# Pooling one pair ahead on GpSimd, and the local mask as an identity product on TensorE

## The chip, the cores and the metric

The kernel runs on one core of one Trainium2 chip. The metric is the time of one execution on the device, in microseconds. The core has TensorE (matrix products into the accumulator banks, PSUM), VectorE, ScalarE, GpSimd (which does not touch PSUM here) and SyncE, whose queue SP issues the loads and stores.

## The reference

Inputs are q, k and v of shape (2, 8, 576, 64), the weights of one feed-forward layer (512 to 2048 to 512) and of four experts (512 to 1024 to 512), and the experts' probabilities for 1152 tokens.

```python
# attention, per batch and head, S = 576, D = 64, factor 4
q_d, k_d, v_d = means over 4 neighbouring positions      # 144 positions
out_up = repeat(softmax(q_d k_d^T / 8) v_d, 4)
mask = abs(i - j) < 4
out_local = softmax(where(mask, q k^T / 8, -1e9)) v
x = (out_up + out_local) as (1152, 512)
h = x @ w_in;  x = (h * sigmoid(h)) @ w_out
p = probs / (probs.sum(-1) + 1e-9)
out = sum over e of p[:, e] * (relu(x @ w1[e]) @ w2[e])
```

## The kernel before, in words

The 16 heads are worked on as N = 8 pairs; the two heads of a pair lie in partitions 0 to 63 and 64 to 127. A software pipeline over `s` runs `step(s)` on each engine; `stage(n, do)` does the part of pair n if it exists. The order within a step is written out by hand for each engine, and semaphores join the engines. A query block has 32 rows (18 blocks a head), and only the window of 38 keys around it is computed: `scores` (L695) makes 36 small products a pair into two banks (`SLB`), `scores_down` (L712) four products of the pooled q and k.

TensorE's step (L766) is: `scores(s)`, `turn_p0(s-1)`, `scores_down(s)`, `values(s-2)`, `turn_p1(s-1)`. The turns (L672, L682; the instructions are at L664 and L669) transpose the probabilities, `values` (L723; L736 local, L743 pooled) multiplies them by v. `warm(count)` (L659) issues transposes whose result nobody reads, ahead of and within the first steps.

VectorE's step (L585): the mask is added to the local scores in place, in PSUM (`mask_scores`, L527, L533), then the row maximum (L537), the subtraction (L542), the pooled maximum (L549), the sums and the normalisation (`norm_local`, L552, which writes `pl` at L565; `norm_down`), and `final(s-2)`, which writes the pair's result `xf`. ScalarE's step (L431) moves the turned probabilities out of PSUM (`evac_p1`, `evac_pd`, `evac_p0`), takes the exponentials (`exp_local` L401, `exp_down`), copies the pooled output (`evac_up`, L421), rounds a pair's result to `x_hi` (`x_high`, L427) and a unit of weights to `wa_hi` (`split_hi`, L366).

GpSimd's step (L327): `down_qk(s)` (L294) adds neighbours of q and k, for q at L300 and L305, for k at L309 and L312; `down_v(s-1)` (L282) does it for v; `x_low` (L314) and `low_unit` (L319) make the rests of x and of a weight unit, `x_lo` and `wa_lo`. `scores(n+1)` needs `pl` of pair n, since it writes the banks that pair n's scores held; `scores_down(n)` needs `qd` and `kd` of pair n; `down_qk` of a pair needs that `scores_down` of the one before has read them.

SP's step (L233) loads q and k of pair s+1 (after `scores` and the pooling of pair s-1), v of pair s, the windows of v of pair s-1 (after `values` of pair s-3), and at s = 0, 1, 3 and 5 a unit of weights. `EARLY` (L179) says in which step a unit is split into its two parts.

After the pairs come the two layers, each product as three (high by high, high by low, low by high) with the data of the two parts. Layer one's first tiles (L757, L796) already run between the last pairs' `values`.

Of the kernel before, what the change touches and what calls it, by code (L numbers as in the profile page):

```python
# [14 lines left out]
P = 128  # L15
# [10 lines left out]
def program(nc, qk, vw, vr, w, probs, out, dims):  # L26
# [31 lines left out]
    with ExitStack() as ctx:  # L58
# [117 lines left out]
            if 0 <= n < N:  # L176
                do(n)

        EARLY = {1: 0, 2: 1, 3: 2, N: 3}  # L179
        XHALF = N // 2  # L180

        def x_of(x, n):
# [21 lines left out]
        @block.sync  # L204
        def _(sp):
            def load_qk(n):
                if n >= 2:
                    sp.wait_ge(s_full, n - 1)
                    sp.wait_ge(qkd_ready, 2 * n - 2)
                sp.dma_start(qk_raw[:, n % 2, :], qk[n]).then_inc(qk_in[n % 2], 16)  # L210

            def load_v(n):
                if n >= 2:
                    sp.wait_ge(vd_ready, n - 1)
                sp.dma_start(v_raw[:, n % 2, :, :, :].rearrange("p a r d -> p (a r d)"), vr[n])\
                    .then_inc(v_in[n % 2], 16)

            def load_win(n):
                if n >= 2:
                    sp.wait_ge(pv_done, n - 1)  # L220
                for h in range(2):
                    sp.dma_start(v_win[HS * h:HS * h + ROWS, n % 2, :, :].rearrange("p g d -> p (g d)"), vw[n, h])\
                        .then_inc(vw_in[n % 2], 16)

            def load_unit(slot, src):
                sp.dma_start(w_raw[:, slot, :], src).then_inc(raw_in[slot], 16)

            def early_unit(u):
                if u >= RAW:
                    sp.wait_ge(w_ready, u - RAW + 1)  # L230
                load_unit(u % RAW, w[u])

            def step(s):  # L233
                stage(s + 1, load_qk)
                stage(s, load_v)
                stage(s - 1, load_win)
                if s in (0, 1):
                    early_unit(s)
                if s in (3, 5):
                    early_unit((s + 1) // 2)  # L240
                if s == 3:
                    sp.dma_start(pr[:, :, :].rearrange("p t e -> p (t e)"), probs).then_inc(pr_in, 16)

            load_qk(0)
            for s in range(N + 1):
                step(s)
            with sp.Fori(2, (FT1 + E * FT2) // RAW) as i:
                for s in range(RAW):
                    u = i * RAW

                    sp.wait_ge(w_ready, u + s - RAW + 1)
                    load_unit(s, w[bass.ds(u + s, 1)].rearrange("o p n -> p (o n)"))
            with sp.Fori(0, T // P) as t:

                sp.wait_ge(out_done, t + (E * (T // P) + 1))
                sp.dma_start(out_v[bass.ds(t, 1)].rearrange("o p d -> p (o d)"),
                             o_acc[:, bass.ds(t, 1), :].rearrange("p o d -> p (o d)")).then_inc(pr_in, 16)
            sp.wait_ge(pr_in, 16 * (1 + T // P))

        @block.gpsimd  # L260
        def _(pool):
# [63 lines left out]
                                   ALU.subtract).then_inc(w_ready, 1)  # L325

            def step(s):  # L327
                stage(s, down_qk)
                stage(s - 1, down_v)
                if s - 4 in range(XHALF):  # L330
                    x_low(s - 4)
                if s in EARLY:
                    u = EARLY[s]
                    low_unit(u + 1, slice(u, u + 1), areas[0], u % RAW)

            for s in range(N + 1):
                step(s)

            def low_units(u0, area, skip=0):
# [22 lines left out]
        def _(act):  # L362
# [68 lines left out]
            def step(s):  # L431
                if s == N + 1:
                    hidden1(0, 0)
                stage(s - 2, evac_p1)
                stage(s - 2, evac_pd)
                stage(s - 1, evac_p0)
                stage(s, exp_local)
                stage(s, exp_down)
                if s == N:
                    act.wait_ge(tick_set, 1)  # L440
                    act.activation(tick[:, 3:4], tick[:, 0:1], ACT.Silu)
                if s == N + 1:
                    hidden1(1, 1)
                stage(s - 2, evac_up)
                if s - 4 in range(XHALF):
                    x_high(s - 4)
                if s in EARLY:
                    split_hi(EARLY[s])

# [52 lines left out]
        def _(dve):  # L502
            dve.memset(ident[:, :], 0.0).then_inc(zeroed, 1)
            dve.memset(band[:, :], 0.0).then_inc(zeroed, 1)
            dve.memset(pl[:, :, :, 0, W:HS], 0.0).then_inc(zeroed, 1)
            odd = GQ * (G % QP)
            dve.memset(ps[odd:P, SLB:SLB + 2, (GT - 1) * W:LC], 0.0).then_inc(zeroed, 1)
            DSTEPS = 5

            def own(n, k):  # L510
                return n * DSTEPS + k
# [12 lines left out]
            def scores_view():  # L524
                return local_scores(0, LC).rearrange("p h (t j) -> p h t j", j=W)

            def mask_scores(n):  # L527
                dve.wait_ge(s_full, n + 1)
                if n == 0:
                    dve.wait_ge(mask_set, QP + 2)  # L530
                    dve.wait_ge(zeroed, 4)
                m = mask[:, :, :].rearrange("p t j -> p (t j)").unsqueeze(1).to_broadcast([P, 2, LC])
                dve.tensor_tensor(local_scores(0, LC), local_scores(0, LC), m, ALU.add).then_inc(dve_step, 1)  # L533

            def max_local(n):
                dve.wait_ge(dve_step, own(n, 1))
                dve.tensor_reduce(mx[:, :].rearrange("p (h t) -> p h t", h=2), scores_view(), AX.X, ALU.max)\  # L537
                    .then_inc(dve_step, 1)

            def sub_max(n):  # L540
                dve.wait_ge(dve_step, own(n, 2))
                dve.tensor_tensor(scores_view(), scores_view(), per_score(mx), ALU.subtract).then_inc(sub_done, 1)  # L542

            def max_down(n):
# [7 lines left out]
            def norm_local(n):  # L552
                par = n % 2
                dve.wait_ge(exp_done, n + 1)
                total = ps[:, SLB, LC:LC + 2 * GT]
                dve.tensor_reduce(total.rearrange("p (h t) -> p h t", h=2), scores_view(), AX.X, ALU.add)\
                    .then_inc(dve_step, 1)
                dve.wait_ge(dve_step, own(n, 3))
                dve.tensor_scalar(rse[:, :], total, EPS, None, ALU.add).then_inc(dve_step, 1)
                dve.wait_ge(dve_step, own(n, 4))  # L560
                dve.reciprocal(rr[:, :], rse[:, :]).then_inc(dve_step, 1)
                dve.wait_ge(dve_step, own(n, 5))
                if n >= 2:
                    dve.wait_ge(p1_turned, n - 1)
                dve.tensor_tensor(pl[:, par, :, :, 0:W].rearrange("p t h j -> p h t j"), scores_view(), per_score(rr),  # L565
                                  ALU.mult).then_inc(pl_ready, 1)
# [16 lines left out]
                    .then_inc(xf_done, 1)  # L583

            def step(s):  # L585
                stage(s, mask_scores)
                stage(s, max_local)
                stage(s, sub_max)
                stage(s, max_down)
                stage(s, norm_local)  # L590
                stage(s, norm_down)
                stage(s - 2, final)
                if s == N:
                    hidden1(0, 0)
# [63 lines left out]
        def _(pe):  # L658
# [36 lines left out]
            def scores(n):  # L695
                par = n % 2
                pe.wait_ge(qk_in[par], 16 * (n // 2 + 1))
                if n >= 1:
                    pe.wait_ge(pl_ready, n)
                else:  # L700
                    pe.wait_ge(zeroed, 4)
                for g in range(G):
                    t, c = g // QP, g % QP
                    at = t * W
                    for h in range(2):
                        rows = slice(D * h, D * h + D)
                        ins = pe.matmul(ps[GQ * c:GQ * c + GQ, SLB + h, at:at + W],
                                        qk_raw[rows, par, GQ * g:GQ * g + GQ],
                                        qk_raw[rows, par, S + GQ * g:S + GQ * g + W], start=True, stop=True)
                ins.then_inc(s_full, 1)  # L710

            def scores_down(n):  # L712
# [48 lines left out]
            def in1(blk, f):  # L761
                layer_in(tile1(blk, f), blk, f, *areas[f // HALF], f)

            WARM = (8, 3, 6, 5, 3)

            def step(s):  # L766
                if s == N + 1:
                    in1(0, 1)
                stage(s, scores)
                if s == 0:  # L770
                    warm(WARM[1])
                stage(s - 1, turn_p0)
                stage(s, scores_down)
                if s < 2:
                    warm(WARM[2 + s])
                stage(s - 2, values)
                if s == N:
                    pe.wait_ge(xlo_done, XHALF)
                    pe.wait_ge(expd_done, 4 * N)
                    in1(0, 0)  # L780
                stage(s - 1, turn_p1)
# [102 lines left out]
```

## Time and profile before

| | us |
|---|---|
| median of 3 runs | 710.99 (710.86 to 712.01) |
| the profiled execution | 711.14 |
| its span, first to last instruction | 709.3 |
| TensorE busy | 685.5 (97%) |
| VectorE, ScalarE, GpSimd busy | 199.5, 163.4, 163.8 |
| `scores` of pair 0 and of pair 7 start at | 4.21 and 75.51 |
| end of the last `values` | 102.53 |

The page cuts the span into 40 slices of 17.7 us; digits are the busy share in tenths, and PEclk is the granted clock in tenths of full speed. Durations of matmuls are modelled at their end, so the distance between the starts of two blocks is the better price of a block. A group's line in the timeline gives start, length, engine, line and operation, shapes and count, and in brackets the idle time before it and what ended that.

### The profile page before, as it was taken

Reading aid. Unit: us, or ns where it says so; the run is one execution under the profiler, and the core shown is the slowest. Engines: PE = TensorE matmul, PEld = TensorE weight load, DVE = VectorE, ACT = ScalarE, POOL = GpSimd, SP = SyncE. Lnnn points to the kernel's source line nnn. Section 1 sums busy time; section 2 is a strip of 40 time slices with the busy share of each in tenths; the row PEclk is TensorE's granted clock in tenths of the full one; section 3 lists DMA queues with packets and bytes.
Section 4 is the critical chain, followed back from the end, with each engine's and each line's share of the span. In section 5 each row is a group of like instructions: output and inputs, shape, how many; then the busy total and the mean of one; then the engine's idle time right before and its main releaser. Section 6 shows DMA issues by size and latency. Waiting matters only on the chain.

```text
span 709.3 us, 11721 instructions
## 1 busy us (share of the span) xinstructions
PE 685.5 (97%) x4574; PEld 635.2 (90%) x4574; DVE 199.5 (28%) x348; ACT 163.4 (23%) x337; POOL 163.8 (23%) x115
## 2 busy tenths in 40 slices
PE   7788899899999999999999999999999999999997
PEld 5577799899999999998989899999999998989896
DVE  7445426733222322221212212121212121212211
ACT  4344443322111213343101042111241111101010
POOL 4636437750000004556000064000262000000000
PEclk9555569999999999999999999999999999999999
DMA  9544213330000001334000033000040000001001
GB/s 272 135 125 132 70 55 119 120 119 1 0 1 1 0 0 65 131 100 149 30 0 0 0 119 118 0 0 0 28 149 0 0 0 0 0 0 44 18 27 44
DMA packets 11227, 38.58 MB, mean 54 GB/s; under 512 B 1536, under 2 KB 1536, under 8 KB 11200
## 3 DMA queue, kind: packets, MB, share of 16 engines
q1 hardware_dynamic: 11200, 38.19, 17.0%
q8 instruction: 20, 0.33, 0.2%
q14 instruction: 7, 0.06, 0.0%
HBM read 35.83 MB, written 2.36 MB: 54 GB/s over the span
## 4 chain that ended last, share of the span: by engine, by line
PE 85%; issue 7%; POOL 5%; DMA 1%; DVE 1%; ACT 0%; DVEq 0%; POOLq 0%; SPq 0%; ACTq 0%
PE ps L757 41%; PE ps L812 28%; PE ps L796 13%; PE ps L736 1%; POOL v L287 1%; POOL x_lo L316 1%; POOL wa_lo L323 1%; POOL k L309 1%; POOL vd L292 1%; POOL q L300 1%; DMA qk_raw<-qk 0%; DMA w_raw<-w 0%; PE ps L743 0%; POOL qd L305 0%; DVE g_lo L601 0%
## 5 line engine op out<-in xcount | busy, mean ns | idle before, releaser
L623 DVE SCALAR_TENSOR_TENSOR g_lo<-ps,g_hi 128x384 fp32r<-128x384 f32 x96 | 53.5, 558 | 270.5 <-ACT g_hi L461 270.5
L461 ACT ACTIVATE g_hi<-ps 128x384 fp32r<-128x384 f32 x96 | 47.1, 491 | 299.8 <-PE ps L757 299.7
L323 POOL TENSOR_TENSOR wa_lo<-w_raw,wa_hi 128x1024 f32 (+1 forms) x24 | 57.3, 2393 | 240.5 <-ACT wa_hi L364 240.4
L757 PE MATMUL ps<-x_hi,wa_hi 128*128 (+1 forms) x288 | 97.4, 338 | 0.0
L757 PE MATMUL ps<-x_hi,wb_hi 128*128 (+1 forms) x288 | 97.2, 337 | 0.0
L757 PE MATMUL ps<-x_lo,wb_hi 128*128 (+1 forms) x288 | 97.1, 337 | 0.0
L757 PE MATMUL ps<-x_hi,wa_lo 128*128 (+1 forms) x288 | 97.1, 337 | 0.0
L757 PE MATMUL ps<-x_hi,wb_lo 128*128 (+1 forms) x288 | 97.0, 337 | 0.0
L757 PE MATMUL ps<-x_lo,wa_hi 128*128 (+1 forms) x288 | 96.9, 336 | 0.0
L323 POOL TENSOR_TENSOR wb_lo<-w_raw,wb_hi 128x1024 f32 x24 | 57.8, 2416 | 104.8 <-ACT wb_hi L364 104.6
L599 DVE CAST g_hi<-g_act 128x384 fp32r<-128x384 f32 x48 | 29.9, 622 | 120.6 <-ACT g_act L456 120.6
L812 PE MATMUL ps<-wa_hi,g_lo 128*128 128x512 f32 x144 | 56.7, 394 | 0.0
L812 PE MATMUL ps<-wb_hi,g_lo 128*128 128x512 f32 x144 | 56.7, 394 | 0.0
L812 PE MATMUL ps<-wa_lo,g_hi 128*128 128x512 f32 x144 | 56.7, 394 | 0.0
L812 PE MATMUL ps<-wb_lo,g_hi 128*128 128x512 f32 x144 | 56.4, 391 | 0.0
L757 PEld LDWEIGHTS ps<-x_hi,wa_hi 128*128 128x128 f32 x288 | 54.6, 190 | 1.9 <-issue 0.4
L812 PE MATMUL ps<-wb_hi,g_hi 128*128 128x512 f32 x144 | 56.3, 391 | 0.0
L812 PE MATMUL ps<-wa_hi,g_hi 128*128 128x512 f32 x144 | 56.0, 389 | 0.0
L757 PEld LDWEIGHTS ps<-x_lo,wa_hi 128*128 128x128 f32 x288 | 54.5, 189 | 1.5
L757 PEld LDWEIGHTS ps<-x_lo,wb_hi 128*128 128x128 f32 x288 | 54.2, 188 | 1.6
L757 PEld LDWEIGHTS ps<-x_hi,wb_hi 128*128 128x128 f32 x288 | 54.3, 189 | 1.4
L757 PEld LDWEIGHTS ps<-x_hi,wa_lo 128*128 128x128 f32 x288 | 54.4, 189 | 0.0
(95 smaller groups left out, 969.4 us busy)
## 6 DMA issues: line engine op xcount, KB each, us to landing
w_raw<-w SPq DMA_DIRECT2D x48, 512.0 KB, 3.5
qk_raw<-qk SPq DMA_DIRECT2D x8, 579.0 KB, 4.5
v_win<-vw SPq DMA_DIRECT2D x16, 216.0 KB, 3.9
v_raw<-vr SPq DMA_DIRECT2D x8, 288.0 KB
out<-o_acc SPq DMA_DIRECT2D x9, 256.0 KB, 2.0
pr<-probs SPq DMA_DIRECT2D x1, 18.0 KB, 4.4
```

The costliest lines, as they stand in the source:

```text
L287: pool.tensor_tensor(v2[:, :, :, :], v_raw[:, par, :, 0:2, :], v_raw[:, par, :, 2:4, :], ALU.add)\
L292: pool.tensor_tensor(vd[:, par, :, :], v2[:, :, 0, :], v2[:, :, 1, :], ALU.add).then_inc(vd_ready, 1)
L300: pool.tensor_tensor(q2[:, :], qv[:, :, 0], qv[:, :, 1], ALU.add).then_inc(qk2_done, 1)
L309: pool.tensor_tensor(k2[:, :], kv[:, :, 0], kv[:, :, 1], ALU.add).then_inc(qk2_done, 1)
L316: pool.tensor_tensor(x_of(x_lo, n), xf[:, n, :], x_of(x_hi, n).bitcast(F32), ALU.subtract).then_inc(xlo_done, 1)
L323: pool.tensor_tensor(lo[:, at, :].rearrange("p o n -> p (o n)"), w_raw[:, s, :], hi[:, at, :].rearrange("p o n -> p (o n)").bitcast(F32), ...
L461: act.activation(g_hi[:, f % GB, :], ps[:, HB + f % 4, 0:NB], ACT.Relu).then_inc(relu_done, 1)
L599: dve.tensor_copy(g_hi[:, f % GB, :], g_act[:, f % 2, :]).then_inc(ghi_done, 1)
L623: dve.scalar_tensor_tensor(out=g_lo[:, f % GB, :], in0=ps[:, HB + f % 4, 0:NB], scalar=0.0, in1=g_hi[:, f % GB, :].bitcast(F32), op0=ALU.m ...
L757: ins = pe.matmul(dst, w[:, f % HALF, c], x[:, kt, at], start=(kt == 0 and i == 0), stop=(kt == KT - 1 and i == 2))
L796: ins = pe.matmul(ps[:, ACCB + j, 0:NB], w[:, f % HALF, c], g[:, f % GB, :], start=(f == 0 and i == 0), stop=(f == FT1 - 1 and i == 2))
L812: ins = pe.matmul(ps[:, ACCB + j, 0:DM], g[:, f % GB, c], w[:, f % HALF, KT * P:UNIT], start=(f == 0 and i == 0), stop=(f == FT2 - 1 and i ...
```

## The change

GpSimd pools pair 0 ahead of the loop and pair s+1 in step s; its loop has one step more, and its `low_unit` of `EARLY` comes one step later than ScalarE's `split_hi`. `EARLY` has step 4 where it had 3, and SP loads these units in steps 4 and 6. ScalarE rounds a pair's result one step earlier. TensorE starts each pair's local scores with two products of the identity by the mask (128 x 190, one for each head's bank), which open the accumulation; the 36 small products add to it. VectorE's mask pass and the memset of the unused part of the banks are gone. In TensorE's step `scores_down(s)` comes ahead of `turn_p0(s-1)`, and the counts of warm-up transposes grow.

```diff
-        EARLY = {1: 0, 2: 1, 3: 2, N: 3}
+        EARLY = {1: 0, 2: 1, 4: 2, N: 3}
...
-                if s in (3, 5):
-                    early_unit((s + 1) // 2)
+                if s in (4, 6):
+                    early_unit(s // 2)
...
             def step(s):
-                stage(s, down_qk)
+                stage(s + 1, down_qk)
                 stage(s - 1, down_v)
                 if s - 4 in range(XHALF):
                     x_low(s - 4)
-                if s in EARLY:
-                    u = EARLY[s]
+                if s - 1 in EARLY:
+                    u = EARLY[s - 1]
                     low_unit(u + 1, slice(u, u + 1), areas[0], u % RAW)
 
-            for s in range(N + 1):
+            down_qk(0)
+            for s in range(N + 2):
                 step(s)
...
-                if s - 4 in range(XHALF):
-                    x_high(s - 4)
+                if s - 3 in range(XHALF):
+                    x_high(s - 3)
...
-            odd = GQ * (G % QP)
-            dve.memset(ps[odd:P, SLB:SLB + 2, (GT - 1) * W:LC], 0.0).then_inc(zeroed, 1)
-            DSTEPS = 5
+            DSTEPS = 4
...
-            def mask_scores(n):
-                dve.wait_ge(s_full, n + 1)
-                if n == 0:
-                    dve.wait_ge(mask_set, QP + 2)
-                    dve.wait_ge(zeroed, 4)
-                m = mask[:, :, :].rearrange("p t j -> p (t j)").unsqueeze(1).to_broadcast([P, 2, LC])
-                dve.tensor_tensor(local_scores(0, LC), local_scores(0, LC), m, ALU.add).then_inc(dve_step, 1)
-
             def max_local(n):
-                dve.wait_ge(dve_step, own(n, 1))
+                dve.wait_ge(s_full, n + 1)
...
                 if n >= 1:
                     pe.wait_ge(pl_ready, n)
                 else:
-                    pe.wait_ge(zeroed, 4)
+                    pe.wait_ge(mask_set, QP + 2)
+                for h in range(2):
+                    pe.matmul(ps[:, SLB + h, 0:LC], ident[:, :], mask[:, :, :].rearrange("p t j -> p (t j)"),
+                              start=True, stop=False, skip_group_check=True)
...
                                         qk_raw[rows, par, GQ * g:GQ * g + GQ],
-                                        qk_raw[rows, par, S + GQ * g:S + GQ * g + W], start=True, stop=True)
+                                        qk_raw[rows, par, S + GQ * g:S + GQ * g + W], start=False, stop=True,
+                                        skip_group_check=True)
...
-            WARM = (8, 3, 6, 5, 3)
+            WARM = (12, 4, 12, 8, 5)
 
             def step(s):
                 if s == N + 1:
                     in1(0, 1)
+                if s == 2:
+                    warm(WARM[4])
                 stage(s, scores)
                 if s == 0:
                     warm(WARM[1])
-                stage(s - 1, turn_p0)
                 stage(s, scores_down)
                 if s < 2:
                     warm(WARM[2 + s])
+                stage(s - 1, turn_p0)
                 stage(s - 2, values)
```

## Rows read from the trace of the kernel before

**Rows 1.** The page: granted clock in 40 slices.

```profile
PEclk9555569999999999999999999999999999999999
```

**Rows 2.** Busy time by stretch: stretch, length, engines, clock, DMA share, GB/s.

```profile
15.56:29.11 13.55, 9.73 (x174) 8.08 (x174) 6.78 (x15) 5.94 (x20) 6.42 (x7) 0.57 0.53 137
53.36:64.43 11.07, 9.75 (x174) 8.20 (x173) 5.69 (x12) 4.54 (x18) 5.43 (x8) 0.50 0.59 168
75.51:87.31 11.80, 9.82 (x174) 8.20 (x174) 5.69 (x12) 5.16 (x19) 6.16 (x8) 0.50 0.22 58
```

**Rows 3.** TensorE's waits up to 103 us: total, times, longest.

```profile
PE ps L719 <- POOL kd L312: 11.8, 6, 2.6
```

**Rows 4.** Timeline of TensorE, pair 6's step.

```profile
64.44 1.08 PE L707 MATMUL ps<-qk_raw 64*32 64x38 f32 x72
65.45 1.09 PE L664 MATMUL ps<-ident,pl 128*102 128x128 f32 x4
67.86 1.24 PE L719 MATMUL ps<-kd,qd 64*72 64x144 f32 x8 [1.32 <-POOL kd L312]
69.03 4.05 PE L736 MATMUL ps<-plT,v_win 38*64 38x32 f32 x72
73.01 1.23 PE L743 MATMUL ps<-pdT,vd 72*64 72x144 f32 x8
74.16 0.46 PE L664 MATMUL ps<-ident,pl 128*102 128x128 f32 x1
75.51 0.44 PE L707 MATMUL ps<-qk_raw 64*32 64x38 f32 x24
```

**Rows 5.** Timeline of GpSimd in the same step.

```profile
64.14 1.41 POOL L316 TENSOR_TENSOR x_lo<-xf,x_hi 128x576 fp32r<-128x576 f32 x1 [5.40 <-ACT x_hi L364]
67.38 0.42 POOL L312 TENSOR_TENSOR kd<-k 128x144 f32<-128x144 f32 x1
```

**Rows 6.** Timeline of TensorE: blocks at the higher clock.

```profile
33.84 0.72 PE L719 MATMUL ps<-kd,qd 64*72 64x144 f32 x8 [2.63 <-POOL kd L312]
34.49 0.74 PE L736 MATMUL ps<-plT,v_win 38*64 38x32 f32 x10
...
96.81 0.27 PE L664 MATMUL ps<-ident,pl 128*102 128x128 f32 x1
...
97.38 0.42 PE L757 MATMUL ps<-x_hi,wa_hi 128*128 128x384 f32 x1
...
99.67 2.29 PE L736 MATMUL ps<-plT,v_win 38*64 38x32 f32 x72
101.88 0.71 PE L743 MATMUL ps<-pdT,vd 72*64 72x144 f32 x8
102.53 0.47 PE L796 MATMUL ps<-g_hi,wa_hi 128*128 128x384 f32 x1
```

**Rows 7.** Timeline of VectorE: the mask pass.

```profile
65.55 0.56 DVE L533 TENSOR_TENSOR ps<-ps,mask 128x380 f32<-128x380 f32 x1 [1.27 <-PE ps L707]
```

**Rows 8.** Timeline of TensorE and ScalarE in step 1.

```profile
11.77 1.24 PE L719 MATMUL ps<-kd,qd 64*72 64x144 f32 x8
14.17 0.67 PE L669 MATMUL ps<-ident,pd 72*72 72x72 f32 x8
15.59 0.35 PE L707 MATMUL ps<-qk_raw 64*32 64x38 f32 x26 [0.76 <-DVE pl L565]
...
13.32 0.47 ACT L404 ACTIVATE ps<-ps 128x380 f32<-128x380 f32 x1 [0.85 <-DVE ps L542]
```

**Rows 9.** Busy time by stretch: at two changes of the granted clock.

```profile
31.20:31.40 0.20, 0.01 (x1) 0.00 (x0) 0.17 (x1) 0.15 (x1) 0.20 (x1) 1.00 0.67 123
102.60:102.80 0.20, 0.20 (x1) 0.20 (x2) 0.00 (x0) 0.16 (x1) 0.00 (x0) 1.00 0.00 0
102.80:103.00 0.20, 0.20 (x2) 0.20 (x2) 0.04 (x1) 0.20 (x2) 0.00 (x0) 0.50 0.00 0
```

**Rows 10.** The chain that ended last, from 95 us: its piece after the last values.

```profile
102.64 0.03 ACT up L364
```

More of the change, by code:

```diff
@@ L525, in scores_view, with max_local @@
                 return local_scores(0, LC).rearrange("p h (t j) -> p h t j", j=W)
-            def mask_scores(n):
+            def max_local(n):
                 dve.wait_ge(s_full, n + 1)
-                if n == 0:
-                    dve.wait_ge(mask_set, QP + 2)
-                    dve.wait_ge(zeroed, 4)
-                m = mask[:, :, :].rearrange("p t j -> p (t j)").unsqueeze(1).to_broadcast([P, 2, LC])
-                dve.tensor_tensor(local_scores(0, LC), local_scores(0, LC), m, ALU.add).then_inc(dve_step, 1)
-            def max_local(n):
-                dve.wait_ge(dve_step, own(n, 1))
                 dve.tensor_reduce(mx[:, :].rearrange("p (h t) -> p h t", h=2), scores_view(), AX.X, ALU.max)\
@@ L540, in sub_max @@
             def sub_max(n):
-                dve.wait_ge(dve_step, own(n, 2))
+                dve.wait_ge(dve_step, own(n, 1))
                 dve.tensor_tensor(scores_view(), scores_view(), per_score(mx), ALU.subtract).then_inc(sub_done, 1)
@@ L557, in norm_local @@
                     .then_inc(dve_step, 1)
+                dve.wait_ge(dve_step, own(n, 2))
+                dve.tensor_scalar(rse[:, :], total, EPS, None, ALU.add).then_inc(dve_step, 1)
                 dve.wait_ge(dve_step, own(n, 3))
-                dve.tensor_scalar(rse[:, :], total, EPS, None, ALU.add).then_inc(dve_step, 1)
+                dve.reciprocal(rr[:, :], rse[:, :]).then_inc(dve_step, 1)
                 dve.wait_ge(dve_step, own(n, 4))
-                dve.reciprocal(rr[:, :], rse[:, :]).then_inc(dve_step, 1)
-                dve.wait_ge(dve_step, own(n, 5))
                 if n >= 2:
@@ L585, in step @@
             def step(s):
-                stage(s, mask_scores)
                 stage(s, max_local)
```

## The prediction

> **What bounds the kernel now.** I read the page first: one core, a span of 709.3 us, 711.14 with what lies around it, and a granted TensorE clock that is low in slices 5 to 9 alone [rows 1]. From about 130 us on TensorE is full at the higher level, and the change does not touch that part. So the question is the attention, up to the last `values` product near 102.5 us.
>
> I then cut the attention at the starts of `scores`, with a view of busy time by stretch [rows 2]. A step is one pair of heads. Pair 2's takes 13.55 us, pair 5's 11.07 us, pair 7's 11.80 us up to the turn at 87.31. In pair 5's step TensorE is busy 9.75 us of 11.07, VectorE 5.69, GpSimd 5.43, all at clock 0.50, the lower of TensorE's two levels (1.2 GHz; the higher is 2.4). TensorE bounds the step, and it has a hole.
>
> The view of waits names the hole: `scores_down` waited for GpSimd's pooling of k, 11.8 us in 6 waits, at most 2.6 [rows 3].  The timeline of one step shows why [rows 4, 5]: GpSimd does `x_low` first, whose `x_hi` copy stands in ScalarE's queue behind `evac_up`, the end of the previous pair's `values`; only then it pools, until 67.80, while TensorE could have started at 66.4. With `low_unit` (2.4 us) in the place of `x_low` (1.41) the hole is 2.6 us.
>
> The prices of TensorE's blocks follow from the starts in this step, at the lower level [rows 4]: `scores` 65.45 - 64.44 = 1.01; `turn_p0` 1.0; `scores_down` 69.03 - 67.86 = 1.17; `values`, local part, 73.01 - 69.03 = 3.98, pooled part 74.16 - 73.01 = 1.15; `turn_p1` 75.51 - 74.16 = 1.35. Sum 9.66. At the higher level the same blocks are [rows 6]: `scores_down` 34.49 - 33.84 = 0.65; `values` 101.88 - 99.67 = 2.21 and 102.53 - 101.88 = 0.65; `turn_p1` 97.38 - 96.81 = 0.57; `turn_p0` half of 1.0, estimated 0.5. `scores` is 72 tiny products whose rate I hold for the same at both levels, 1.0. Sum 5.6. So the clock is worth 4.1 us a step, three times the hole.
>
> **The change, part by part.** *Pooling ahead.* GpSimd pools pair s+1 in step s, after `scores_down(s)` has read `qd` and `kd`. Its work in a step is 5.43 us [rows 2], and `x_low` now takes an `x_hi` that ScalarE wrote a step before, so GpSimd waits for nothing late. SP's load of pair n, which waited for the pooling of n-2, may go earlier; the loads of v and of its windows keep their waits. One more pair of `low_unit` moves goes with it; they stay beside TensorE. Gain: the hole, 2.6 us in steps 2 to 4 and 1.3 in 5 to 7, all of it. What would be late next is TensorE's own work.
>
> *The mask.* VectorE loses one pass, 0.56 us and its gap, 0.6 us [rows 7], which lies in the chain from `scores` to `pl` and not on TensorE's path after step 2. TensorE gains two products of 128x128 by 190 columns per pair, in fp32, each issued as two instructions. None is in the trace. The nearest rows are `scores_down`, eight instructions of 144 columns in 1.17 us. If the two row halves (h = 0, 1) run beside each other, one instruction has 0.29 us for 144 columns, and the mask's four cost 4 x 0.29 x 190/144 = 1.5 us; if they run in turn it is 0.77. Four transposes of 128 columns in 1.0 us give 4 x 0.25 x 190/128 = 1.5 too, so I take 1.5 at the lower and 0.8 at the higher level, with 0.77 as the low end and, should the identity's loads not hide (four loads near 0.17 us), 2.2 as the high end. All of it is on the path. With it a step of TensorE's is 9.66 + 1.5 = 11.15 us at the lower level and 5.6 + 0.8 = 6.4 at the higher. So if the clock stays, the mask eats what the pooling gives in steps 5 to 7 (11.07 before): the change lives by the clock. The dropped VectorE memset lies in TensorE's warm-up and costs nothing either way; the new wait for `mask_set` ends at about 3.4 us, before the q and k load lands at 4.2.
>
> *The order.* `turn_p0(s-1)` goes behind `scores_down(s)`. On ScalarE `evac_p0(s-1)` waits for it, and `exp_local(s)` stands behind that, then VectorE's sums and `pl`, for which `scores(s+1)` waits. From the exponential's start to the next `scores` it is 15.59 - 13.32 = 2.3 us [rows 8]. At the higher level `pl` is there at 0.8 + 1.0 + 0.65 + 0.5 + 0.7 (evacuation) + 2.3 = 5.95 us, just inside 6.4; at the lower at 7.7 of 11.15. Covered, except in steps 0 and 1, which have no `values` to cover it.
>
> *Steps 0 and 1, and the warm-up products.* Twelve transposes at 0.25 us end at 4.6 instead of before 4.21, the mask ends at 6.1, `scores(0)` at 7.1 against 5.2, less VectorE's 0.6: step 1 would start 1.3 us later at the lower level, less if the clock has risen; I take 0.8 later, 10.5. In step 1 the exponential waits for mask, `scores`, `scores_down`, eight warm products, `turn_p0` and the evacuation: 6.65 + 0.7 + 2.3 = 9.7 us at the lower, 7.0 at the higher level, against 5.85 before. I take 8.0: step 2 starts at 18.5 instead of 15.56. Loss 2.9 us.
>
> The duration rows tell more of this start than the clock column, which says 1.00: `scores_down` takes 1.24 us at 11.77, as at the lower level, and the turn of eight tiles 0.67 at 14.17, as at the higher [rows 4, 6, 8]. So the clock rose only near 14 us, and fell before 20.
>
> *The clock.* In the old kernel it stood at 1.00 at 31.2 us, after slices at half speed [rows 1, 9], right after `turn_p1`, `scores` and `turn_p0` had run without a hole. It fell at 102.8 with TensorE busy all through both sides [rows 9]: behind it lay `values`, small tiles. The new step holds both kinds: `turn_p1`, mask, `scores`, `scores_down`, `turn_p0` in one block of 1.35 + 1.5 + 1.0 + 1.2 + 1.0 = 6 us with the densest product of all in it, then 5 us (2.9 at the higher level) of `values`. So I expect a rise in the first half of every step and a fall in or after the second, and take the mean of the two prices: (11.15 + 6.4) / 2 = 8.8 us.
>
> Sum: 18.5 + 6 x 8.8 = 71.3 us for the turn of pair 7, against 87.31: 16 us less. What follows (15.2 us to the end of the last `values`, then a chain that begins with that pair's `up` copy at 102.64 [rows 10]) is the same work in the same order and moves as a whole. Against the profiled execution's 711.14: 711.1 - 16.0 = 695.1. The median of the runs shown is 710.99, so the same forecast holds for it.
>
> The Trainium skill's page "TensorE: Matmul & The Clock Gate", section on PE-mode transpose, says that transposes do not count as busy for the clock. By that the warm products would be worth nothing, steps 0 and 1 would run at the lower level, step 2 would start at 21.3 and the sum would be 698. The rows speak against it: the rise near 14 us came after turns, `scores_down` and five warm transposes.
>
> **Rivals.** *A: the clock rises and stays (chance 0.11).* For it: no hole is left. Against: the fall at 102.8 with TensorE busy. Steps of 6.4 us from 17.0: 55.4 at pair 7's turn, 31.9 us less, and some 3 more from the tail: 676. The same page's practical advice has the clock fall back for idle gaps alone; by that rule the new kernel would do just this.
>
> *B: the clock stays low; the mask on TensorE is the new bound (0.13).* For it: in the old trace it stayed at 0.50 through all of pairs 5 to 7 with 9.75 of 11.07 us busy [rows 2], and TensorE was without a hole from 67.86 to 76.5 [rows 4]. Against: the rise near 31. Step 2 starts at 21.3, six steps of 11.15 end at 88.2, 0.9 later than 87.31: 712. The mask's price decides: at 0.77 us it would be 706, at 2.2 some 717; above 1.35 us this rival is slower than before. This is the case on the other side.
>
> *The forecast (0.76)* has its own range from the share of a step at the higher level: 8.8 +- 1.2 us, 688 to 702.
>
> **Numbers.** 0.2% is 1.4 us, about what a measurement of this kernel can tell from no change. The forecast and A are faster (0.87); B is split by the mask's price, 0.08 slower, 0.04 within, 0.01 faster. The range 680 to 709 leaves out most of A below and B's upper half above, some 2 in 10.
>
> **What would show it.** `scores_down` waits for GpSimd no more; two new products of 190 columns stand ahead of `scores`, some 0.75 us each at the lower level; the line of VectorE's mask is gone; steps of 8 to 10 us with the clock changing inside each, `values` some times 2.2 us and some times 4. Pair 7's turn near 71 us, and the work from there on unchanged. I am wrong if the steps are above 10 us (B), below 7 (A), or if a new wait stands on TensorE: for `pl` after step 1, or for a load of q and k.

## The result and the profile after

The changed kernel takes 693.68 us (median of 4 runs, 692.11 to 694.59) against 710.92 for the kernel before, a ratio of 0.9752 with a 95% interval of 0.9728 to 0.9776. The forecast was 695. A second comparison on another chip gave 693.61 and 0.9744 (0.9716 to 0.9773). The runs of the changed kernel scatter by up to six us, those of the kernel before by up to three, apart from one execution beside experiments 1 to 4 that took 842.6 us at a mean clock of 0.73, a slow state that is not compared.

The profiled execution took 694.59 us, its span is 692.7. The page, which answers to [rows 1]:

```profile
span 692.7 us, 11813 instructions
PEclk9857899999999999999999999999999999999999
```

The low digits are fewer and uneven: the clock now changes inside the attention. The view of busy time by stretch, cut at the start of each pair's first mask product, pair 2 to pair 7, answers to [rows 2] (columns as there: stretch, length, TensorE, its weight loads, VectorE, ScalarE, GpSimd, clock, DMA share, GB/s):

```profile
16.33:22.66 6.33, 6.33 (x178) 5.45 (x178) 5.52 (x13) 4.80 (x17) 4.80 (x8) 1.00 0.63 151
22.66:33.48 10.82, 8.65 (x181) 7.35 (x178) 9.97 (x12) 5.06 (x18) 8.41 (x9) 0.77 0.75 186
33.48:44.52 11.04, 11.04 (x179) 9.31 (x178) 8.51 (x13) 4.47 (x17) 7.14 (x9) 0.50 0.70 192
44.52:52.88 8.36, 8.36 (x180) 6.91 (x178) 4.26 (x8) 4.83 (x17) 4.30 (x6) 0.70 0.43 120
52.88:62.81 9.93, 9.10 (x179) 7.69 (x178) 9.32 (x14) 4.70 (x18) 9.59 (x10) 0.67 0.65 157
62.81:71.47 8.66, 7.80 (x180) 6.49 (x178) 6.37 (x13) 4.55 (x18) 4.58 (x5) 0.81 0.29 73
```

Here both of my bounds stand as whole steps: 6.33 us with the clock high throughout (forecast 6.4), 11.04 with it low throughout (forecast 11.15), TensorE without a hole in either. The others lie between. VectorE's column is new as well: 5.69 to 6.78 us a step before, up to 9.97 now, with no more instructions.

TensorE's largest waits up to 90 us, in place of [rows 3]:

```profile
PE ps L693 <- DVE pl L556: 2.2, 2, 1.2
PE ps L700 <- issue: 2.2, 1, 2.2
...
PE ps L654 <- ACT pdT L365: 0.9, 1, 0.9
PE ps L730 <- DVE xf L573: 0.8, 1, 0.8
```

The 11.8 us of waiting for GpSimd's pooled k are gone. The waits for `pl` end steps 0 and 1. The one called issue (the engine waited for nothing that the profile shows) is a hole in pair 3's step, and the one for `xf`, in pair 6's, is new.

The timeline of TensorE, first pair 1, then pair 4's step, gives the price of the product that [rows 4] could not show:

```profile
9.78 0.88 PE L693 MATMUL ps<-mask,ident 128*128 128x190 f32 x4 [0.99 <-DVE pl L556]
10.60 0.84 PE L700 MATMUL ps<-qk_raw 64*32 64x38 f32 x72
11.37 0.71 PE L713 MATMUL ps<-kd,qd 64*72 64x144 f32 x8
...
33.48 1.57 PE L693 MATMUL ps<-mask,ident 128*128 128x190 f32 x4
34.98 1.08 PE L700 MATMUL ps<-qk_raw 64*32 64x38 f32 x72
35.98 1.24 PE L713 MATMUL ps<-kd,qd 64*72 64x144 f32 x8
```

From start to start the product takes 0.82 us at the higher level and 1.50 at the lower; `scores` takes 0.77 and 1.00.

The last pair's `up` copy, the head of the chain after the attention, stood at 102.64 [rows 10] and is now, in the chain that ended last, here:

```profile
86.11 0.03 ACT up L365
```

That is 16.5 us earlier, and the span is 16.6 us shorter. All of the gain is in the attention, and what follows moved as a whole.

### The profile page after: what moved, and what is told of

Same layout as the page of the kernel before. It is cut to its first block, busy times and chain, and to the rows that moved or that the text cites. A ratio compares the mean times of both kernels' runs of the same rounds, so it can differ in the third digit from the quotient of the medians.

```text
span 692.7 us, 11813 instructions
## 1 busy us (share of the span) xinstructions
PE 677.3 (98%) x4625; PEld 628.9 (91%) x4625; DVE 207.3 (30%) x339; ACT 162.2 (23%) x337; POOL 165.1 (24%) x115
## 4 chain that ended last, share of the span: by engine, by line
PE 93%; DVE 2%; POOL 2%; issue 1%; ACT 1%; DMA 0%; DVEq 0%; POOLq 0%; SPq 0%; ACTq 0%
PE ps L751 42%; PE ps L808 29%; PE ps L792 13%; PE ps L730 3%; PE ps L693 1%; PE ps L654 1%; PE ps L737 1%; POOL x_lo L316 1%; PE ps L700 1%; PE ps L713 1%; POOL wa_lo L323 1%; PE ps L651 1%; PE ps L659 1%; DVE rsde L562 1%; DMA w_raw<-w 0%
```

## The experiments

Each was run beside the kernel before, and ratios are to it. Line numbers are those of each kernel's own file.

**1. The mask back on VectorE, all else of the change kept.** The pass and the memset come back, the product goes.

```diff
-                for h in range(2):
-                    pe.matmul(ps[:, SLB + h, 0:LC], ident[:, :], mask..., start=True, stop=False, ...)
...
-                ... start=False, stop=True, skip_group_check=True)
+                ... start=True, stop=True)
...
+                stage(s, mask_scores)
                 stage(s, max_local)
```

> The changed kernel with the mask back on VectorE and the identity product gone; all else of the change stays. Theory (the dense product is what lifts the clock): TensorE's step is 9.66 us at the lower level and 5.6 at the higher, but the clock rises in fewer steps; steps of about 9 us, pair 7's turn near 73 us, some 695 to 698 us, no faster than the changed kernel. Rival (the product is only a cost, the clock alternates without it): steps of (9.66 + 5.6) / 2 = 7.6 us, 686 to 688 us.

Measured: 693.45 us (691.68 to 694.49), 0.9742 (0.9718 to 0.9767): the same as the changed kernel. The rival's 686 to 688 is out. The theory's main point holds, that taking the product away makes the kernel no faster, though its time was 2 to 4 us too long.

**2. The pooling ahead alone.** The kernel before, with this, the longer loop and the later weight units:

```diff
-                stage(s, down_qk)
+                stage(s + 1, down_qk)
...
-                if s in EARLY:
-                    u = EARLY[s]
+                if s - 1 in EARLY:
+                    u = EARLY[s - 1]
...
+            down_qk(0)
...
-                if s - 4 in range(XHALF):
-                    x_high(s - 4)
+                if s - 3 in range(XHALF):
+                    x_high(s - 3)
```

> The kernel before with only the pooling ahead (and what goes with it on SP, ScalarE and in GpSimd's loop); old order, old warm-up, mask on VectorE. Theory: the hole goes in all six steps, at least 12 us saved, 697 to 699 if the clock stays low and about 690 if it rises in every other step. Rival (the hole was a symptom, another wait takes its place): over 705.

Measured: 696.67 us, 0.9793 (0.9775 to 0.9810), and no wait for the pooled k is left. A pair's step from its timeline of TensorE, up to the next one's `scores`:

```profile
26.88 1.08 PE L708 MATMUL ps<-qk_raw 64*32 64x38 f32 x72
27.89 1.09 PE L665 MATMUL ps<-ident,pl 128*102 128x128 f32 x4
28.91 1.24 PE L720 MATMUL ps<-kd,qd 64*72 64x144 f32 x8
30.08 4.05 PE L737 MATMUL ps<-plT,v_win 38*64 38x32 f32 x72
34.06 1.23 PE L744 MATMUL ps<-pdT,vd 72*64 72x144 f32 x8
...
36.56 0.69 PE L708 MATMUL ps<-qk_raw 64*32 64x38 f32 x38
```

The step is 36.56 - 26.88 = 9.68 us, the 9.66 of [rows 4] with the hole cut out, all at the lower level. The pooling by itself carries 2.1% of the 2.5%. Between this kernel and that of experiment 1, run beside the same kernel before, lie only the order of the turns and the warm-up counts, and the intervals are apart (696.67 and 693.45 us). So what the change gives beyond the pooling is there without the mask product.

**3. The mask product alone.** The kernel before, with VectorE's pass and the memset gone and the two products in `scores`.

```diff
+                for h in range(2):
+                    pe.matmul(ps[:, SLB + h, 0:LC], ident[:, :], mask[:, :, :].rearrange("p t j -> p (t j)"),
+                              start=True, stop=False, skip_group_check=True)
...
-                stage(s, mask_scores)
```

> The kernel before with only the mask as an identity product on TensorE, VectorE's pass gone; GpSimd pools as before. Theory: the product, 1.50 us at the lower level, goes ahead of scores, while GpSimd's chain is what TensorE waits for in scores_down; the hole of 1.3 to 2.6 us hides most of it, and the clock rises more often: 705 to 711. Rival (the product lies on the path and the clock does not follow): 6 x 1.5 less the holes, over 713.

Measured: 704.29 us, 0.9909 (0.9880 to 0.9938), a little faster than I had allowed. Its TensorE waits less for the pooled k, though the longest wait is 3.2 us, not 2.6:

```profile
PE ps L712 <- POOL kd L312: 6.8, 4, 3.2
```

6.8 us instead of 11.8 [rows 3]: the product fills part of the hole, and the mean granted clock from 20 to 70 us is 0.67 instead of 0.53. Parts 2 and 3 add up to 3.0%, the whole change gives 2.5%, which the intervals hardly tell apart. With the hole gone the product gives nothing more: experiment 1.

**4. The old counts of warm-up transposes.**

```diff
-            WARM = (12, 4, 12, 8, 5)
+            WARM = (8, 3, 6, 5, 3)
```

> The changed kernel with the old counts of warm-up transposes (8, 3, 6, 5, 3). Theory: the clock is at the higher level from about 5 us in the changed kernel; with fewer transposes it rises later or falls within steps 0 to 2, which costs 2 to 5 us: 695 to 699. Rival (the transposes do not count for the clock and only fill time): no difference or up to 1 us faster, 692 to 694.

Measured: 695.04 us, 0.9771 (0.9742 to 0.9800). The centre is where the theory had it, but the interval overlaps the changed kernel's. In its profile `scores_down` of pair 0 already runs at the higher level (7.57 to 8.25 us), where the old kernel's took 1.24 us at 6.04; in the changed kernel the higher level stands at `scores` of pair 0, 5.25 us. That is not the counts alone: in the first profile of experiment 8, with the same step 0 as the changed kernel, `scores` still takes 1.02 us at 5.76.

**5. Transposes among the values products.**

```diff
                 for turn_over in range(2):
+                    for _ in range(3):
+                        pe.transpose(ps[:, OUTB, 3 * P:4 * P], ident[:, :], ident[:, :])
                     for i in range(G // 2):
```

> The changed kernel with 2 x 3 transposes of the identity (128 columns each, result unread) among each pair's local values products. They cost 1.5 us a step at the lower and 0.8 at the higher level. Theory (it is the small tiles of values that let the clock fall, TensorE busy or not): the clock stays high through most steps, 6.4 + 0.8 = 7.2 us a step, pair 7's turn near 60 us, 682 to 687. Rival (the fall has another cause): the transposes are pure cost, 7 or 8 pairs by 1.15, some 701 to 703.

Measured: 698.03 us, 0.9807 (0.9786 to 0.9828). Neither number came. Three transposes take 0.42 to 0.47 us at the higher level in its timeline, so six in each of eight pairs cost at least 7 us, and about 4 are seen (the intervals allow 1.6 to 6.2). A part comes back, and by the time alone it cannot be said whether from the clock.

**6. The mask product twice.**

```diff
-                for h in range(2):
+                for h in (0, 1, 0, 1):
                     pe.matmul(ps[:, SLB + h, 0:LC], ident[:, :], mask...
```

> The changed kernel with the mask product issued twice per bank (the second overwrites the first with the same values). Theory (the product pays for itself in clock): of the 1.5 or 0.8 us more a step a good part comes back, 694 to 699. Rival (pure cost): 8 pairs by 1.15 us, 702 or more.

Measured: 695.55 us (692.17 to 697.13), 0.9768 (0.9731 to 0.9806). Pure cost is out: at least 0.64 us more per pair at the higher level and 1.26 at the lower, eight times, would be 5 to 10 us, and 2 are seen (the intervals allow up to 4.3).

**7. The mask product in bf16.**

```diff
-        mask = asb("mask", [P, GT, W])
+        mask = sb("mask", [P, GT, W], BF16, att)
+        ident16 = sb("ident16", [P, P], BF16, att)
...
-                    pe.matmul(ps[:, SLB + h, 0:LC], ident[:, :],
+                    pe.matmul(ps[:, SLB + h, 0:LC], ident16[:, :],
```

> The changed kernel with mask and identity in bf16 for the mask product, one instruction instead of two for each bank; 0 and the large negative value are as good in it. The product should cost at most 0.4 us a pair at the lower level instead of 1.50. Theory (what is saved in columns is lost in clock): 690 to 695, as with the mask on VectorE. Rival (pure cost): 1.1 us at the lower, 0.6 at the higher level saved, 685 to 688.

Measured: 694.28 us, 0.9785 (0.9740 to 0.9830). In the timeline the cheap product takes 0.45 us at the lower and 0.26 at the higher level, against 1.50 and 0.82, and the kernel gains nothing by it. Its view of busy time over three steps points to why:

```profile
26.00:56.00 30.00, 29.90 (x524) 25.23 (x526) 21.81 (x35) 13.90 (x49) 20.56 (x23) 0.50 0.68 173
```

TensorE is busy 29.90 us of 30 and is granted 0.50 all the time. The changed kernel in the same stretch:

```profile
26.00:56.00 30.00, 29.57 (x538) 24.90 (x539) 22.45 (x33) 13.82 (x49) 20.38 (x23) 0.60 0.64 164
```

It is no busier, and has more clock; the bf16 kernel of experiment 10 has 0.50 in this stretch as well. What the two differ in is the product, dense and long in the one and short in the other. The granted clock from 20 to 70 us, in the same view, through kernels with less and more of it. Pooling ahead only:

```profile
20.00:70.00 50.00, 48.84 (x948) 41.49 (x947) 44.77 (x68) 25.75 (x92) 37.66 (x39) 0.57 0.58 149
```

Mask on VectorE:

```profile
20.00:70.00 50.00, 45.87 (x892) 38.10 (x888) 43.63 (x68) 26.21 (x94) 37.08 (x40) 0.62 0.65 167
```

The changed kernel:

```profile
20.00:70.00 50.00, 47.00 (x945) 39.71 (x942) 39.14 (x61) 24.98 (x92) 35.80 (x38) 0.69 0.61 154
```

Transposes among the values products:

```profile
20.00:70.00 50.00, 46.21 (x907) 38.41 (x903) 37.59 (x55) 22.46 (x81) 35.41 (x38) 0.76 0.60 154
```

The product twice:

```profile
20.00:70.00 50.00, 44.62 (x1063) 38.64 (x1063) 38.74 (x62) 25.43 (x91) 37.20 (x40) 0.90 0.63 159
```

The first profile of experiment 8, which has the same dense product as the changed kernel:

```profile
20.00:70.00 50.00, 44.25 (x987) 36.88 (x986) 35.67 (x65) 26.78 (x97) 36.50 (x40) 0.82 0.68 166
```

In this view the two kernels without the product have 0.57 and 0.62, the two with it in bf16 (experiments 7 and 10) 0.66 and 0.63, and the seven with one fp32 product between 0.67 and 0.82. The transposes among the `values`, at 0.76, are inside that spread; the product twice, at 0.90, is above it. TensorE's busy time lies between 43.85 and 48.84 us in all of them and does not order them.

These are single profiles. The mean clock over the whole execution is known for every run, and orders the kernels alike:

| | runs | mean clock, lowest to highest |
|---|---|---|
| pooling ahead only (experiment 2) | 4 | 0.949 to 0.966 |
| mask on VectorE (1) | 4 | 0.956 to 0.968 |
| product in bf16 (7, 10) | 9 | 0.949 to 0.968 |
| changed kernel, both times | 10 | 0.964 to 0.980 |
| `final` first, both times (8) | 9 | 0.966 to 0.983 |
| old order (9) | 5 | 0.962 to 0.980 |
| old warm-up counts (4) | 4 | 0.926 to 0.973 |
| transposes among the `values` (5) | 4 | 0.975 to 0.978 |
| product twice (6) | 4 | 0.981 to 0.985 |

The product alone with the old pooling (experiment 3) has 0.953 to 0.966, where the kernel before has mostly 0.936 to 0.945. The attention is an eighth of the execution, so the differences are small: by my estimate 0.01 is 14 us (0.02 of 691) more or less at the lower level. Not every one of these means fits its time (three runs of the kernel before have 1.00 at 711 to 713 us), so only groups count.

**8. VectorE's `final(s-2)` ahead of `norm_down(s)`.** The new wait for `xf` led here. In the changed kernel's timeline of VectorE and of GpSimd, pair 5's step:

```profile
51.99 3.72 DVE L562 TENSOR_SCALAR rsde<-rsd 72x4 f32<-72x4 f32 x1
...
55.96 0.97 DVE L566 TENSOR_TENSOR pd<-pd,rrd 72x576 f32<-72x576 f32 x1
56.85 0.74 DVE L573 TENSOR_TENSOR xf<-ps,up 128x576 f32<-128x576 f32 x1
...
51.97 1.41 POOL L316 TENSOR_TENSOR x_lo<-xf,x_hi 128x576 fp32r<-128x576 f32 x1
53.34 2.35 POOL L323 TENSOR_TENSOR wa_lo<-w_raw,wa_hi 128x1024 fp32r<-128x1024 f32 x1
```

An addition on 72 x 4 values, 0.17 us in the old kernel, takes 3.72: it begins as GpSimd's `x_low` does and ends with its `low_unit`. In pair 2's step it is the `pd` product, 3.47 us instead of 0.75. VectorE's `xf` stands behind them, and `values` waits for `xf`.

```diff
-                stage(s, norm_down)
-                stage(s - 2, final)
+                stage(s - 2, final)
+                stage(s, norm_down)
```

> The changed kernel with VectorE's final(s-2) ahead of norm_down(s). In the changed kernel the pd product of norm_down takes up to 3.47 us beside GpSimd's two-input work (0.75 alone), final stands behind it, and values once waited 0.83 us for xf. Theory: that wait goes, and with it 1 to 3 us: 690.5 to 693. Rival (the wait only moves, to pd for turn_p1): 693 to 695.

Measured: 691.84 us, 0.9720 (0.9692 to 0.9748); the wait for `xf` is gone from its profile. Since this touches the changed kernel's 0.9752 (0.9728 to 0.9776), it was run again, with the changed kernel beside it:

> The changed kernel itself, for a comparison on one chip with the next three. 692 to 695, ratio 0.973 to 0.977.

> Once more VectorE's final(s-2) ahead of norm_down(s). If the wait of values for xf is a real cost (0.8 us in the changed kernel's profile, 1.4 to 2.6 us in those of its variants), this is 1 to 3 us faster than the changed kernel beside it; if what was seen (691.8) was the scatter of the clock, there is no difference.

Measured: 693.61 us and 0.9744 (0.9716 to 0.9773) for the changed kernel, 691.85 and 0.9712 (0.9691 to 0.9734) with `final` first. In the changed kernel's profile of this comparison the waits of TensorE have this line, and the other has none for `xf`:

```profile
PE ps L730 <- DVE xf L573: 2.6, 1, 2.6
```

Twice 1.8 us faster, with intervals that overlap each time: likely better than both kernels, and clearly better than the one before, but the step from the changed kernel is not proved. The wait is partly replaced: holes called issue add up to 5.1 and 2.9 us with `final` first, against 2.2 and 2.7 in the changed kernel.

**9. The old order of `turn_p0` and `scores_down`.**

```diff
+                stage(s - 1, turn_p0)
                 stage(s, scores_down)
                 if s < 2:
                     warm(WARM[2 + s])
-                stage(s - 1, turn_p0)
```

> The changed kernel with turn_p0(s-1) ahead of scores_down(s) again, as in the kernel before. Theory (pl is covered after step 1, so the order only matters in steps 0 and 1): exp_local of pair 1 starts about 2 us earlier, but the eight warm-up transposes then stand behind it; within 1.5 us of the changed kernel. Rival (the order keeps the dense products together and carries the clock): 3 us or more slower.

Measured: 694.42 us, 0.9761 (0.9737 to 0.9784): no difference that this resolves. The order is worth nothing measurable.

**10. `final` first and the bf16 product.**

> final(s-2) first and the mask product in bf16. Theory (columns saved are lost in clock): as the one with final first, 690 to 693. Rival (with the wait gone the cheaper product counts): 686 to 689.

Measured: 695.53 us, 0.9784 (0.9762 to 0.9807), against 0.9712 for the same kernel with the fp32 product, and the intervals are apart. I had expected no difference; the product that takes TensorE a fraction of the time makes the kernel 3.7 us slower. The mean clock is 0.953 to 0.965 in its five runs and 0.966 to 0.983 in the five with the fp32 product: no overlap. Its profile has the clock low from 22.8 to 56.6 us. The profiles themselves compare badly, since this one is its kernel's fastest run (693.23 us) and the other's is its slowest (696.30). Neither the start (pair 0's product at 4.21 us) nor the holes called issue (2.7 against 2.9 us) explain the time. This is the cleanest evidence that the dense columns pay in clock.

## Why the prediction was right

- *Where.* The low clock stands in the second to sixth of the 40 slices of [rows 1], 17.7 to 106 us, not in "slices 5 to 9"; the prediction's own times fit the former, and nothing else hangs on the slip.
- *The hole.* All of it went, as forecast; what came late next was mostly TensorE's own work. Experiment 2 shows the step at 9.68 us against the 9.66 of the sum. I had left out that the pooling ahead makes GpSimd's work fall together with VectorE's.
- *The product's price.* 1.50 us at the lower level (forecast 1.5), 0.82 at the higher (0.8). That is the bound for two row halves of `scores_down` beside each other; in turn would have been 0.77.
- *Steps of 8.8 us.* The six take 71.47 - 16.33 = 55.1 us, 9.2 each. The 8.8 was too short by two holes that I did not have: 2.2 us in pair 3's step and 0.8 for `xf`. Without them the mean is 8.7.
- *Steps 0 and 1.* Forecast to lose 2.9 us; pair 2 starts at 16.33 instead of 15.56, a loss of 0.8. The clock rose before 5.3 us, not near 14 as in the kernel before, and `scores` is not the same at both levels, 0.77 against 1.00. This error of 2.2 us offset the 2.3 us of the steps, so pair 7's turn is at 71.47 where 71.3 was forecast. The close agreement is in part luck. Rival B's start of step 2, 21.3 us, does not follow from its terms either: 9.7 + 1.3 + 9.7 is 20.7, so its 712, and the 698 of the sum with worthless transposes, are 0.6 too long.
- *The tail.* From that turn to the end of the last `values` 14.5 us against 15.2, at a mean clock of 0.76 against 0.72; beyond it nothing changed.
- *The order.* Covered, as forecast: experiment 9.
- *The clock.* As forecast in kind: in the six steps it rose at 49.0, 55.9 and 66.1 us, each time behind a pair's mask product and `scores`, and it fell at 28.6, 52.5, 59.3 and, in the next, at 72.9, each time in or right behind a pair's `values`. Not in every step: pair 2's has no fall, pair 4's no rise. Before three of the falls there was a hole of 0.8 us or more within 5 us; before the one at 52.5 there had been none since 26.4. The view of busy time around it:

```profile
52.20:52.40 0.20, 0.20 (x5) 0.20 (x5) 0.20 (x1) 0.20 (x2) 0.20 (x1) 1.00 0.06 23
52.60:52.80 0.20, 0.20 (x5) 0.20 (x3) 0.20 (x1) 0.20 (x1) 0.20 (x1) 0.50 0.00 0
```

Just before lay a pair's `values` and its turn. By the Trainium skill's page "TensorE: Matmul & The Clock Gate", section "Why this matters for your kernels", an engine without long idle gaps should have kept the higher level, rival A; no run did, the nearest being the product issued twice, at 0.90, and experiment 7 was granted 0.50 for 30 us with TensorE busy for 29.90 of them. That page's section on PE-mode transpose would make transposes worthless for the clock. Experiment 5 has 0.76 against 0.69 and 0.76, which does not settle it. The start of experiment 1's trace, where no mask product stands ahead of `scores`, does:

```profile
1.60 2.82 PE L662 MATMUL ps<-ident 128*128 128x128 f32 x12 [1.60 <-POOL ident L263]
4.60 0.85 PE L708 MATMUL ps<-qk_raw 64*32 64x38 f32 x72 [0.18 <-DMA qk_raw<-qk]
5.38 0.66 PE L662 MATMUL ps<-ident 128*128 128x128 f32 x4
```

TensorE had run twelve transposes and nothing else, at the lower level (twelve take 1.53 us at the higher, at 7.26 in the changed kernel), and `scores` takes 5.38 - 4.60 = 0.78 us, as at the higher level. With eight transposes ahead, in the kernel before and in experiment 2, `scores` of pair 0 takes 1.00 and 1.01. So in this kernel transposes do lift the clock, and the measurement decides against the page. How early it rises is not set by the work alone: after the same step 0 on TensorE it was up at 9.80 us in experiment 2 and only near 14 in the kernel before. What the warm-up counts are worth in time is 1.4 us by experiment 4, with an interval from 1.3 less to 4.0 more, and up to 3.2, together with the order, by experiments 1 and 2.
- *Rival B*, the low clock, did not come for the whole, but pair 4's step is it, 11.04 us. My statement that the change lives by the clock was too strong: the pooling alone gives 2.1% at a clock that stays low for most of the attention, since it also cuts the 1.3 us of the later steps where no product is added. What lives by the clock is the mask on TensorE, and it comes out even as nearly as this measures: with it or with the pass on VectorE the time is the same.

## What to carry to other kernels

When the bounding engine is TensorE and its clock is low, price every block at both levels and read which blocks a rise or fall follows; an engine that is never idle can still be granted half its clock if its products are small. A dense product can then cost less than its length, and making it cheaper can cost time, so test such an edit on the chip and not by the sum of durations. And when a stall goes because one engine's work is moved earlier, see what it now runs beside: here the two-input work of GpSimd stretched one of VectorE's small operations twentyfold.

## What the runs showed of the hardware that I had not expected

VectorE's `rsde` went from 0.17 to 3.72 us and the `pd` product from 0.75 to 3.47 while GpSimd worked on two inputs. The Trainium skill's page "GPSIMD Engine Reference", section "Specifications", says that the two engines share their SBUF interfaces, with contention for VectorE instructions with two SBUF inputs or in a two-port mode; the `pd` product, with two inputs, agrees. The small addition has one SBUF tensor as input, and no row says whether it ran in a two-port mode; both waits lasted until the second of two GpSimd instructions had ended.

The profile's clock column says 1.00 for the start of the kernel before, while its blocks run at the lower level's durations until near 14 us. In each profile here the column is only good from the first fall on.

In the attention all kernels but that of experiment 3 have holes in TensorE's work that the profile calls issue, 0.2 to 3.1 us long. Counted with the view of busy time they come after the same numbers of weight loads whatever instruction stands there: 221 (the kernel before and experiment 2), 474 or 475 (nine of the fourteen profiles), 600, 725 or 726, 978, 1103 and 1229. From 475 on these lie some 125 apart or a multiple of it. In the changed kernel the share of the DMA engines is 0.82 to 1.05 in each microsecond of its hole, which would point to the engine's own instructions arriving behind the bulk loads. Two others speak against that as the whole cause: in the first profile of experiment 8 a hole of 1.68 us, after 1103 weight loads, has a DMA share of 0.00, and in its second profile one of 1.37 us, after 1229, has 0.03. The regular count points to how the instructions reach the engine; nothing was run on it, and the cause stays open.
